# Turned tiles of a top-2 expert layer: dense 128-byte moves, rows one step sooner, weight loads on SyncE's queue, one flag per tile

## The chip, the cores and the metric

The kernel runs on one core of a Trainium2 chip. The metric is the device time of one execution in microseconds. The kernel before takes 1312.8 us (median of 3 runs, 1312.21 to 1313.14). A measurement of this kernel can tell a change from none at about 0.2%, some 2.6 us.

## What is computed

A retention-like attention feeds a dense feed-forward layer, and that feeds a layer of 8 experts of which every token takes two. The change touches the expert layer alone:

```python
logits = x @ w_gate
noise_scale = np.log1p(np.exp(x @ w_noise))
noisy_logits = logits + noise_scale * noise
top2 = np.argpartition(-noisy_logits, 2, axis=1)[:, :2]
# top2_w: softmax of the two
for e in range(E):                       # E = 8
    for k in range(2):
        mask = top2[:, k] == e
        h = np.maximum(x[mask] @ w1[e], 0.0)
        out[mask] += top2_w[mask, k, None] * (h @ w2[e])
```

x has 2304 rows of 512, w1[e] is 512x1024, w2[e] is 1024x512, all fp32.

## The kernel before

**Stages.** Attention and the dense layer take the first 500 us or so. During the dense layer the kernel writes, for every expert, a list of its tokens in DRAM. The expert layer then works through these lists in tiles of 128 tokens; in this run there are 41 tiles, 0 to 40, some five per expert. Which expert a tile belongs to is known only at run time: VectorE (DVE) computes two small tables, `tab` and `tab2`, with one column per tile, and every engine reads its numbers from there (`entry` and `entry2`, lines 358 and 362: a load of one value into a register, then register instructions).

**One tile g.** GpSimd (POOL) gathers its 128 rows of x (`xg`), two tiles in flight. They must be transposed for TensorE (PE), as must the hidden values between the two products. Tiles from 2 on are turned without TensorE: VectorE transposes blocks of 32x32 (`turn_x` into `turned_x`, `turn_hidden` into `hid`, in two halves h), and DMAs move each group of 32 partitions to its place (`move_x` into `x_there`, 4 moves of 64 KB; `move_hidden` into `h_there`, 2 times 4 moves of 64 KB). Each move writes 128 runs of 512 bytes. What lands has the elements of a column 4 apart, so that its readers step by 16 bytes (`landed`). ScalarE (ACT) makes the high part of every value (`split_moved`, with the Relu, and `split_moved_x`), VectorE the rest (`split_moved`, `split_moved_x`), since each product is done as three products of parts (`three`, lines 826 to 828).

**TensorE's order** is fixed: `expert_in(g + 1)`, then `expert_out(g)`, then `expert_in(g + 2)`, `expert_out(g + 1)`; each is 24 matmuls of 512 columns, and each waits for the lower parts that VectorE made.

**A step g of the others**, word by word in the code below: ScalarE waits for the rows of tile g+2, loads the row numbers of tile g+4 (`load_meta`), splits hidden(g), splits weights for tile g+1 (w1), splits x(g+2), splits weights for tile g (w2), loads raw weights twice (`load_weights`), and loads the row numbers of output tile g+1 (`next_rows`). VectorE makes the rest of hidden(g), turns x(g+2) and hidden(g+1), makes the rest of x(g+2), and adds the output of tile g (`add_output`). SyncE (SP) moves x(g+2), then hidden(g+1). GpSimd gathers rows of tile g+3 (`gather_x`), the old output rows of tile g (`old_rows`) and scatters the new ones (`send_rows`).

**Weights.** An expert's weights come in four quarters of 1 MB (`raw`), two of w1 and two of w2, and are split into `ew`, which holds two experts. The table says at which tiles a quarter is split (`T_SPLIT`) and loaded (`T_LOAD`): at an expert's first and second tile. So each `split_weights` asks two questions of the table and each `load_weights` two, by a load from `tab2` and a branch over what is left out. ScalarE asks eight times per step, VectorE four times.

**The loops** run over pairs of steps (`Fori`), so every engine jumps back once per two tiles.

## Time and profile of the kernel before

| | us |
|---|---|
| median of 3 runs | 1312.8 |
| the profiled execution | 1312.81 |
| span of its instructions | 1310.8 |
| TensorE busy (matmuls) | 1031.6 |
| VectorE busy | 563.7 |
| ScalarE busy | 446.6 |
| GpSimd busy | 206.6 |
| mean granted TensorE clock | 0.901 |

The page of the profile cuts the span into 40 slices. TensorE is over 90% busy in the first sixteen and between 40% and 80% in nearly all of the rest, which is the expert layer; no other engine is above 70% in any slice there. Starts are counted in us from the start of the span. "ACTq", "SPq", "DVEq" are the queues (sequencers) of these engines: register, branch and DMA-issuing instructions. "issue" is time in which an engine waited for nothing that the profile shows. The chain that ended last is followed back from the last instruction.

### The profile page before, as it was taken

To read this page: it belongs to the slowest core of one execution; us is meant where nothing else is said; L and a number is where in the kernel's file an instruction comes from. 1 tells how busy PE (TensorE), PEld (TensorE's weight loads), DVE (VectorE), ACT (ScalarE), POOL (GpSimd) and SP (SyncE) were. 2 spreads that over 40 slices of the span, in tenths; PEclk is the share of its full clock that TensorE was granted. 3 is DMA by queue.
4 is the path that set the end of the run, shared out by engine and by line. 5 is a ranking of instruction groups with operands and counts; after the bars stand their busy time and mean duration, and the time that the engine had idled before them with its cause. 6 is when DMAs were issued, how large, how long until landed. Compare 5 with 4: busy or idle time off the path is not lost.

```text
span 1310.8 us, 21213 instructions
## 1 busy us (share of the span) xinstructions
PE 1031.6 (79%) x5392; PEld 855.2 (65%) x5393; DVE 563.7 (43%) x919; ACT 446.6 (34%) x649; POOL 206.6 (16%) x198
## 2 busy tenths in 40 slices
PE   9999999999999999676777746665375577787764
PEld 8889989898989887555555635453354455565553
DVE  4665243333425466433333624464353444433342
ACT  2367555555555663111111311232232321111111
POOL 5500001010102023211122011100101112121111
PEclk9999999999999999788899878887778788878888
DMA  9835200000000532633333343344534333333331
GB/s 298 286 124 185 80 1 25 1 24 0 24 0 21 180 109 47 208 82 91 87 87 94 101 131 101 93 141 148 185 102 133 106 79 92 83 83 89 83 73 51
DMA packets 115285, 128.84 MB, mean 98 GB/s; under 512 B 26813, under 2 KB 91709, under 8 KB 111040
## 3 DMA queue, kind: packets, MB, share of 16 engines
q1 hardware_dynamic: 89472, 78.05, 21.0%
q0 software_dynamic: 10992, 27.84, 6.8%
q10 hardware_dynamic: 14688, 21.65, 5.1%
q14 instruction: 108, 0.88, 0.2%
q8 instruction: 25, 0.41, 0.1%
HBM read 81.31 MB, written 20.37 MB: 78 GB/s over the span
## 4 chain that ended last, share of the span: by engine, by line
PE 37%; ACTq 20%; issue 17%; DMA 7%; SPq 6%; DVE 5%; ACT 4%; DVEq 2%; POOL 0%; POOLq 0%
ACTq L362 11%; PE bank L826 11%; PE bank L828 10%; PE bank L827 10%; DMA x_there<-turned_x 6%; SPq L535 5%; ACTq L358 5%; DVE turned_x L1640 3%; ACT hT_hi L1237 3%; ACTq L375 2%; DVEq L362 2%; PE bank L776 1%; PE bank L750 1%; ACTq L379 1%; PE bank L769 1%
## 5 line engine op out<-in xcount | busy, mean ns | idle before, releaser
L826 PE MATMUL bank<-ew,hT_hi 128*128 (+1 forms) x320 | 154.1, 482 | 206.5 <-DVE hT_lo L1660 206.5
L826 PEld LDWEIGHTS bank<-ew,hT_hi 128*128 128x128 f32 x320 | 74.4, 232 | 238.4 <-issue 222.4
L1237 ACT ACTIVATE hT_hi<-h_there 128x512 fp32r<-128x512 f32 x76 | 80.2, 1103 | 353.7 <-issue 342.0
L1660 DVE SCALAR_TENSOR_TENSOR hT_lo<-h_there,hT_hi 128x512 fp32r<-128x512 f32 x76 | 79.0, 1069 | 279.6 <-ACT hT_hi L1237 279.6
L826 PE MATMUL bank<-ew,xgT_hi 128*128 (+1 forms) x328 | 138.6, 422 | 52.0 <-DVE xgT_lo L1654 47.5
L827 PE MATMUL bank<-ew,hT_hi 128*128 (+1 forms) x320 | 146.1, 456 | 0.0
L828 PE MATMUL bank<-ew,hT_lo 128*128 (+1 forms) x320 | 144.3, 451 | 0.0
L827 PE MATMUL bank<-ew,xgT_hi 128*128 (+1 forms) x328 | 134.3, 410 | 0.0
L828 PE MATMUL bank<-ew,xgT_lo 128*128 (+1 forms) x328 | 133.6, 407 | 0.0
L826 PE MATMUL bank<-xs_hi,mw 128*128 128x384 f32 x384 | 129.9, 338 | 0.0
L828 PE MATMUL bank<-xs_hi,mw 128*128 128x384 f32 x384 | 129.5, 337 | 0.0
L827 PE MATMUL bank<-xs_lo,mw 128*128 128x384 f32 x384 | 128.9, 336 | 0.0
L651 POOL DMA_INDIRECT out<-ysb,meta_y x41 | 42.9, 1047 | 534.6 <-DVE ysb L1673 534.6
L826 PEld LDWEIGHTS bank<-ew,xgT_hi 128*128 128x128 f32 x328 | 65.2, 199 | 81.3 <-issue 68.4
L1413 DVE SCALAR_TENSOR_TENSOR act_t<-bank,act_t 128x384 f32<-128x384 f32 x90 | 50.2, 558 | 150.7 <-ACT act_t L1153 149.8
L826 PE MATMUL bank<-mw,g_hi 128*128 128x512 f32 x288 | 114.6, 398 | 0.0
L828 PE MATMUL bank<-mw,g_lo 128*128 128x512 f32 x288 | 113.7, 395 | 0.0
L827 PE MATMUL bank<-mw,g_hi 128*128 128x512 f32 x288 | 113.4, 394 | 0.0
L1243 ACT ACTIVATE xgT_hi<-x_there 128x512 fp32r<-128x512 f32 x38 | 42.3, 1114 | 205.6 <-DMA x_there<-turned_x 205.6
L619 POOL DMA_INDIRECT lists<-rec,slot x36 | 35.6, 990 | 379.1 <-DVE slot L1512 370.0
L828 PEld LDWEIGHTS bank<-ew,hT_lo 128*128 128x128 f32 x320 | 73.3, 229 | 18.2
L827 PEld LDWEIGHTS bank<-ew,hT_hi 128*128 128x128 f32 x320 | 74.6, 233 | 15.8
(233 smaller groups left out, 1624.6 us busy)
## 6 DMA issues: line engine op xcount, KB each, us to landing
raw<-w_ex ACTq DMA_DIRECT2D x20, 1024.0 KB, 4.9
h_there<-hid SPq DMA_DIRECT2D x312, 64.0 KB
raw<-w_ex SPq DMA_DIRECT2D x12, 1024.0 KB, 5.1
x_there<-turned_x SPq DMA_DIRECT2D x152, 64.0 KB, 2.1
stage<-w_ff SPq DMA_DIRECT2D x16, 512.0 KB, 3.4
out<-blank SPq DMA_DIRECT2D x3, 1536.0 KB, 11.1
x_rows<-x2sb SPq DMA_DIRECT2D x6, 768.0 KB, 4.4
kbuf<-kN SPq DMA_DIRECT2D x16, 256.0 KB, 4.1
```

Of the source, the lines that this page charges most:

```text
L358: return eng.value_load(tab[row:row + 1, bass.ds(g, 1)], min_val=low, max_val=high)
L362: return eng.value_load(tab2[row:row + 1, bass.ds(g, 1)], min_val=low, max_val=high)
L535: sp.dma_start(x_there[:, i * P:(i + 1) * P], turned_x[32 * i:32 * i + 32, :].rearrange("a (j n) -> a j n", j=4)).then_inc(x_moved, 16)
L651: pool.indirect_dma_start(out=out[:, :], out_offset=rows, in_=ysb[:, s, :], in_offset=None, bounds_check=N - 1, oob_is_err=False).then_inc ...
L826: pe.matmul(o, a_hi, b_hi, start=first, stop=False)
L827: pe.matmul(o, a_hi, b_lo, start=False, stop=False)
L828: return pe.matmul(o, a_lo, b_hi, start=False, stop=last)
L1237: nc.scalar.activation(h_hi[:, 4 * h:4 * h + 4, :], landed(h_there[:, h, :]), ACT.Relu).then_inc(hT_hi_done, 1)
L1243: nc.scalar.activation(xgT_hi[:, s, :, :], landed(x_there[:, :]), ACT.Copy).then_inc(xgT_hi_done, 1)
L1413: dve.scalar_tensor_tensor(t, h_ps[f % 4], 0.0, t, ALU.max, ALU.add).then_inc(g_done, 1)
L1640: dve.transpose(turned_x[:, :].rearrange("p (j b c) -> p j c b", j=4, b=32), xg[:, s, :].rearrange("p (c a j) -> p j c a", j=4, a=32)).the ...
L1660: dve.scalar_tensor_tensor(h_lo[:, k, :], landed(h_there[:, h, :]), 0.0, as32(h_hi[:, k, :]), ALU.max, ALU.subtract).then_inc(hT_lo_done, 1)
```

## The change

Six edits, all in the expert layer.

- **Layout.** The turned tiles are laid out so that a move writes dense runs: `h_there` and `x_there` are now [128, tiles of 128 columns, 128], a move fills 32 of every 128 columns (runs of 128 bytes), and the readers read them without a step. VectorE's transposes write contiguous runs of 32.
- **Moves.** Hidden is moved in 4 moves of 128 KB (each 128 x 8 x 32) instead of 8 of 64 KB, after both halves are turned, under one semaphore. x is still moved in 4 of 64 KB (128 x 4 x 32).
- **Rows one step sooner.** VectorE turns x(g+3) at the end of step g, not x(g+2) near its beginning, and SyncE moves it behind hidden(g+1).
- **Weight loads** leave ScalarE's queue for SyncE's, behind the moves of the step.
- **One flag per tile** (`T_BUSY`, the larger of the two split flags): one question in front of each pair of splits and each pair of loads. The two questions behind it are asked only where the flag is set.
- **ScalarE's order.** Hidden(g) is split first, and the wait for rows and the load of row numbers come after.

```diff
-        h_there, a = place("h_there", [P, 2, 4 * P], F32, a)
-        x_there, a = place("x_there", [P, 4 * P], F32, a)
+        h_there, a = place("h_there", [P, FT2, P], F32, a)
+        x_there, a = place("x_there", [P, KT, P], F32, a)
...
-        def landed(ap):
-            return ap.rearrange("p (t c) -> p c t", c=4)
+        def landed(ap, i):
+            return ap[:, :, 32 * i:32 * i + 32]
...
-                    sp.dma_start(x_there[:, i * P:(i + 1) * P], turned_x[32 * i:32 * i + 32, :].rearrange("a (j n) -> a j n", j=4)
+                    sp.dma_start(landed(x_there, i), turned_x[32 * i:32 * i + 32, :].rearrange("a (n b) -> a n b", b=32)
...
-            def move_hidden(g, h):
-                sp.wait_ge(h_turned, g * 2 + h + 1)
+            def move_hidden(g):
+                sp.wait_ge(h_turned, g * 2 + 2)
                 for i in range(4):
-                    sp.dma_start(h_there[:, h, i * P:(i + 1) * P],
-                                 hid[32 * i:32 * i + 32, h * 512:(h + 1) * 512].rearrange("a (j n) -> a j n", j=4)
-                                 ).then_inc(h_moved[h], 16)
+                    sp.dma_start(landed(h_there, i), hid[32 * i:32 * i + 32, :].rearrange("a (n b) -> a n b", b=32)
+                                 ).then_inc(h_moved, 16)
...
+            def move(g, rows=True):
+                move_hidden(g + 1)
+                if rows:
+                    move_x(g + 3)
+                for of, p in (g + 1, 0), (g, 1):
+                    with sp.If(entry2(sp, T_BUSY, of, 0, 1)):
+                        load_weights(sp, of, p)
-            with sp.Fori(1, pair) as i:
+            with sp.Fori(1, prior) as i:
                 for s in range(2):
-                    g = 2 * i + s
-                    move_x(g + 2)
-                    move_hidden(g + 1, 0)
-                    move_hidden(g + 1, 1)
+                    move(2 * i + s)
+            move(2 * prior)
+            move(2 * prior + 1, False)
...
             def split_weights(g, p):
-                for q in range(2):
-                    with act.If(entry2(act, T_SPLIT[q], g, 0, 1)):
+                with act.If(entry2(act, T_BUSY, g, 0, 1)):
+                    for q in range(2):
+                        with act.If(entry2(act, T_SPLIT[q], g, 0, 1)):
...
             def step(i, s):
                 g = 2 * i + s
+                split_moved(g, g)
                 alone(act, got_x[s], i * 16 + 32)
                 load_meta(act, meta_x, s, g + 4, ld_mx[s])
-                split_moved(g, g)
                 split_weights(g + 1, 0)
                 split_moved_x(g + 2, s, g + 1)
                 split_weights(g, 1)
-                load_weights(act, g + 1, 0)
-                load_weights(act, g, 1)
                 next_rows(i, s)
...
-                dve.transpose(turned_x[:, :].rearrange("p (j b c) -> p j c b", j=4, b=32),
+                dve.transpose(turned_x[:, :].rearrange("p (j c b) -> p j c b", j=4, b=32),
...
+            dve.tensor_tensor(col(cols2, T_BUSY), other, goal, ALU.max)
...
             def step(i, s, end=False):
                 g = 2 * i + s
                 split_moved(g)
-                turn_x(g + 2, s, i + 2)
                 turn_hidden(g + 1, 0)
                 split_weights(g + 1, 0)
                 turn_hidden(g + 1, 1)
                 split_moved_x(g + 2, s)
                 split_weights(g, 1)
-                if end:
+                if not end:
+                    turn_x(1 - s, i + s + 2)
+                else:
                     split_moved(g + 1, hE_hi, hE_lo)
                 add_output(i, s)
```

SyncE's queue, kernel before: what stands at the top of its loop over pairs of steps, for the first of the two steps (x of tile g+2, then the two halves of hidden(g+1)).

```order
L561 ISA
L535 DMA x_there<-turned_x 128x1x128 [waits xgT_made]
L535 DMA x_there<-turned_x 128x1x128 x3
L540 ISA
L542 DMA h_there<-hid 128x1x128 [waits h_turned]
L542 DMA h_there<-hid 128x1x128 x3
L540 REGISTER_ALU
L542 DMA h_there<-hid 128x1x128 [waits h_turned]
L542 DMA h_there<-hid 128x1x128 x3
```

SyncE's queue, kernel after, the same place.

```order
L568 ISA
L541 DMA h_there<-hid 128x8x32 [waits h_turned]
L541 DMA h_there<-hid 128x8x32 x3
L532 REGISTER_ALU
L534 DMA x_there<-turned_x 128x4x32 [waits xgT_made]
L534 DMA x_there<-turned_x 128x4x32 x3
L361 ISA
L361 TENSOR_LOAD tab_116
L361 ISA x2
L565 COMPARE_AND_BRANCH
```

Hidden goes first and in half as many moves, x goes second, and behind them stand the flag's load and the branch over the weight loads.

ScalarE's queue, kernel before: from the jump target of its loop on (`hT_hi` is the high part of hidden, `tab_116` is `tab2`).

```order
L1330 ISA
L358 ISA [waits got_x0]
L358 TENSOR_LOAD tab
L358 ISA x2
L375 ISA
L375 DMA meta_x<-lists 128x2
L1236 REGISTER_ALU [waits m2_done]
L1237 ACTIVATE hT_hi<-h_there 128x512 [waits h_moved0]
L1237 ACTIVATE hT_hi<-h_there 128x512 [waits h_moved1]
```

ScalarE's queue, kernel after, the same place.

```order
L1334 ISA
L1241 REGISTER_ALU [waits m2_done]
L1242 ACTIVATE hT_hi<-h_there 128x512 [waits h_moved] x2
L335 ISA
L357 ISA [waits got_x0]
L357 TENSOR_LOAD tab
L357 ISA x2
L374 ISA
L374 DMA meta_x<-lists 128x2
```

The split of hidden stands ahead of the wait for rows.

VectorE's queue, kernel before: the end of one step (the output) and the beginning of the next.

```order
L1673 SCALAR_TENSOR_TENSOR ysb<-bank,meta_y,prev 128x512 [waits sent_y0,got_prev0]
L1658 ISA
L1660 SCALAR_TENSOR_TENSOR hT_lo<-h_there,hT_hi 128x512 [waits hT_hi_done]
L1658 REGISTER_ALU
L1660 SCALAR_TENSOR_TENSOR hT_lo<-h_there,hT_hi 128x512 [waits hT_hi_done]
L1640 STREAM_TRANSPOSE turned_x<-xg 128x4x4x32 [waits got_x1]
L1649 STREAM_TRANSPOSE hid<-bank 128x4x4x32 [waits in_half]
```

VectorE's queue, kernel after, the same place.

```order
L1644 STREAM_TRANSPOSE turned_x<-xg 128x512 [waits got_x1]
L1670 REGISTER_ALU
L1672 REGISTER_ALU [waits m2_done]
L1677 SCALAR_TENSOR_TENSOR ysb<-bank,meta_y,prev 128x512 [waits sent_y0,got_prev0]
L1662 ISA
L1664 SCALAR_TENSOR_TENSOR hT_lo<-h_there,hT_hi 128x512 [waits hT_hi_done]
L1662 REGISTER_ALU
L1664 SCALAR_TENSOR_TENSOR hT_lo<-h_there,hT_hi 128x512 [waits hT_hi_done]
L1653 STREAM_TRANSPOSE hid<-bank 128x4x128 [waits in_half]
```

The turning of x now stands ahead of the output of its step, and the turning of hidden follows its split directly.

## Rows read from the trace of the kernel before

**Rows 1.** Stretches of line L1237: us, ACT busy (count), PEclk, DMA share, GB/s
```profile
575.20:720.00 144.80, 16.89 (x16) 0.88 0.34 87
720.00:1083.20 363.20, 33.78 (x33) 0.80 0.41 120
1083.20:1294.90 211.70, 25.35 (x25) 0.87 0.33 83
```
**Rows 2.** Timeline of ACT: start, us, engine, line, names [idle before <-releaser]
```profile
1228.02 2.11 ACT L1237 ACTIVATE hT_hi<-h_there 128x512 fp32r<-128x512 f32 x2 [10.92 <-issue]
1236.44 1.12 ACT L1243 ACTIVATE xgT_hi<-x_there 128x512 fp32r<-128x512 f32 x1 [6.31 <-DMA x_there<-turned_x]
...
1244.30 2.12 ACT L1237 ACTIVATE hT_hi<-h_there 128x512 fp32r<-128x512 f32 x2 [6.74 <-issue]
```
**Rows 3.** Timeline of DVE, same step
```profile
1229.16 2.08 DVE L1660 SCALAR_TENSOR_TENSOR hT_lo<-h_there,hT_hi 128x512 fp32r<-128x512 f32 x2 [9.43 <-ACT hT_hi L1237]
1231.15 1.14 DVE L1640 STREAM_TRANSPOSE turned_x<-xg 128x512 f32<-128x512 f32 x1
1232.17 1.98 DVE L1649 STREAM_TRANSPOSE hid<-bank 128x512 f32<-128x512 f32 x2
...
1239.85 0.75 DVE L1673 SCALAR_TENSOR_TENSOR ysb<-bank,meta_y,prev 128x512 f32<-128x512 f32 x1 [1.18 <-issue]
```
**Rows 4.** Timeline of SP, same step
```profile
1232.32 2.48 SPq L535 DMA_DIRECT2D x_there<-turned_x  x4
1234.93 5.09 SPq L542 DMA_DIRECT2D h_there<-hid  x8
```
**Rows 5.** Timeline of PE: the first of each three matmuls
```profile
1218.43 0.69 PE L826 MATMUL bank<-ew,xgT_hi 128*128 x1 [2.68 <-DVE xgT_lo L1654]
1219.77 0.63 PE L826 MATMUL bank<-ew,xgT_hi 128*128 x1
...
1238.90 0.49 PE L826 MATMUL bank<-ew,xgT_hi 128*128 x1 [0.33 <-DVE xgT_lo L1654]
...
1243.78 0.39 PE L826 MATMUL bank<-ew,xgT_hi 128*128 x1
```
**Rows 6.** Pieces of the chain at the end of ACT's loop: start, us, what
```profile
1222.07 2.41 issue
...
1224.71 2.12 issue
```
**Rows 7.** Table loads of line L362 in 1228:1264.5: count: duration min/median/max in ns
```profile
L362 ACTq TENSOR_LOAD <-tab x16: 273/278/431, 1228.1 to 1256.5; - x16
```
**Rows 8.** Groups by form (busy us, mean ns), and a split of weights in ACT's timeline
```profile
L1257 ACT ACTIVATE ew<-raw 128x2048 f32 x24 | 45.9, 1914 | 38.7 <-issue 35.3 <-PE bank L828 3.4
L1833 DVE TENSOR_TENSOR ew<-raw,ew 128x2048 f32 x24 | 55.0, 2293 | 42.2 <-ACT ew L1257 42.2
...
963.81 1.92 ACT L1257 ACTIVATE ew<-raw 128x2048 f32 x1 [2.79 <-issue]
```
**Rows 9.** DMA queue 1 in 1230:1243 (moves): packets, MB, share of 16 engines
```profile
q1 hardware_dynamic: 1728, 0.79, 26.7%
```
**Rows 10.** DMA queue 1 in 63.05:63.85: mostly the gate weights' 128-byte runs
```profile
q1 hardware_dynamic: 573, 0.09, 74.7%
```
**Rows 11.** Issues of DMAs of many runs: duration min/median/max in ns
```profile
L477 SPq DMA_DIRECT2D wg<-w_gn x1: 1320/1320/1320, 61.1 to 61.1; - x1
...
L487 SPq DMA_DIRECT2D out<-blank x3: 636/1854/4470, 120.7 to 123.3; - x3
```
**Rows 12.** Instruction queue in 60.8:62.5, and an issue of 128 runs
```profile
q8 instruction: 1, 0.02, 4.4%
...
29.31 1.36 SPq L421 DMA_DIRECT2D qbuf<-qT  x1
```
**Rows 13.** Timeline of POOL
```profile
1224.63 1.01 POOL L645 DMA_INDIRECT prev<-out,meta_y  x1 [1.63 <-issue]
```
**Rows 14.** Page, part 6: gathers of old output rows, us to landing
```profile
prev<-out,meta_y POOLq DMA_INDIRECT x39, 3.4
```

66 lines of the change are left out of this document (33 added, 33 removed).

## The prediction, made before the changed kernel ran

> **What bounds the kernel now.** I read the two halves of the page first: only the expert layer has idle time on TensorE, so the question is what a step of it waits for. The stretches by the starts of ScalarE's split of hidden (two per tile) give the length of a step [rows 1]: 8 steps in 144.8 us and 12 in 211.7 us where no weights are split, together 356.5 / 20 = 17.8 us, and 16 steps in 363.2 us with the 24 quarters of weights (45.9 us at 1.91 [rows 8]). 363.2 - 16 x 17.8 = 78.4, or 3.3 us for each quarter.
>
> A step holds two products of 24 matmuls. At full clock one product runs from 1238.90 to the last triple at 1243.78 and ends 0.68 later: 5.56 us [rows 5]. Two take 11.1 us. So 6.7 of 17.8 us are waits. The timelines show whose. From 1228.02, where ScalarE splits hidden(g), the order is: VectorE's rest of hidden 2.08, turning of x 1.14, turning of hidden 1.98 [rows 3]; SyncE's eight issues for hidden begin only at 1234.93, behind the four for x, and end at 1240.02 [rows 4]; x is split at 1236.44, 1.6 us after the last issue for x had ended (1232.32 + 2.48 = 1234.80) [rows 2, 4]. By the same 1.6 us hidden(g+1) is there at 1241.6. But ScalarE takes it at 1244.30: since the end of x (1237.56) its queue has gone 6.74 us through questions to the table and two loads of row numbers [rows 2]. Sixteen questions are asked in two steps [rows 7]; six of the eight of a step stand in those 6.74 us, with two loads of row numbers, so that one costs about 0.7 us. In the other step of the pair ScalarE jumps back, and there it stands still for 2.41 and 2.12 us [rows 6]. Two limits lie close together, then: ScalarE's queue, and behind it the row VectorE, SyncE, ScalarE. TensorE has to slow down besides: after a wait of 2.68 us a triple takes 1.34 us (1218.43 to 1219.77), not 0.70 [rows 5], at the lower level of the clock.
>
> **The change, part by part**, for a step without weights.
>
> *ScalarE's questions and loads.* Eight questions become two, 6 x 0.7 = 4.2 us less per step. The four load questions and the waits for VectorE in front of weight loads go to SyncE. Hidden is split before the wait for rows and the load of row numbers, some 1.3 us, so these now lie under VectorE's work. Left on ScalarE after hidden: row numbers 1.2, question 0.7, x 0.6, question 0.7, row numbers 1.2; this is 4.4 us. The stall at the jump back, 4.5 us per pair, I keep: 9 us are under 11.1.
>
> *Dense reads.* Now 512 stepped columns take 1.06 us on ScalarE and 1.04 on VectorE [rows 2, 3]. Dense ones take 1914 / 2048 = 0.93 and 2293 / 2048 = 1.12 ns a column [rows 8], 0.48 and 0.57 us, with a fixed part about 0.6 and 0.65. In the row from hidden to hidden this is 0.45 + 2 x 0.4 = 1.2 us; bounds are 0 (if only the step of the write mattered) and 1.3. The Trainium skill, SBUF — State Buffer, Specifications and its note on cachelines, lets fp32 be stepped by up to 4 elements for free; by that the 1.2 us would not come, and the chain below would be 11.2 instead of 10.0. The rows speak against it, at double the time per column.
>
> *x one step sooner.* x(g+2) has landed before its step begins, so the 6.31 us that ScalarE waits for it [rows 2] go, and 1.14 of turning and 2.48 of issues leave the way of hidden [rows 3, 4]. Its rows must be gathered sooner by the same half step. They are asked for right after the output of the tile before is sent, a whole step ahead. I cost this at nothing. The turning now stands ahead of the output of its step and delays that if the gather is late; the old output rows stand ready at 1224.63 + 3.4 = 1228.0 for an addition at 1239.85 [rows 3, 13, 14], so 11.8 us of slack shrink to about 5.
>
> *Moves.* Four issues for hidden instead of eight. What one costs is not shown for this shape: 512-byte runs from 32 to 128 partitions took 2.48 / 4 = 0.62 us [rows 4], 512 runs of 128 bytes 1.32, 1536 runs of 1 KB 0.64 in the first of three [rows 11]. I take 0.62 to 0.7: the issue with 1.32 lies beside a transfer of instructions, and an issue of just 128 runs took 1.36 us elsewhere [rows 12], so 1.32 isn't the price of runs. The upper end is 1.32 for x and twice that for hidden. The data: 1728 packets of the moves took 26.7% of 16 engines for 13 us, 32 ns each [rows 9]; those of 128 bytes at most 0.747 x 800 x 16 / 573 = 16.7 ns [rows 10]. There are 4096 for hidden, 256 per engine, 4.3 us (1024 now, 64 per engine, 2.1 us, hidden behind the issues). At 32 ns it would be 8.2 us. I take 16.7, since that row has the size of the runs. So the transfers get slower, and the issues fewer: landing from the first issue about 1.1 + 4.3 + 0.5 = 5.9 us, against 5.09 + 1.6 = 6.7.
>
> *SyncE's weight loads.* At 1 MB each they queue behind the moves of their step and ahead of the next hidden, more than 8 us later. SyncE also waits there for VectorE's rest of the quarter, but x, in front of it, was turned behind both splits, so this wait is over. Behind it stands the next hidden. Nothing, while SyncE has 11.1 us and uses 2.5 + 2.5 + 1.4 plus its own jump back (bounded by ScalarE's 4.5).
>
> *The sum.* From the start of VectorE's rest of hidden(g): 1.4 + 1.98 turning + 5.9 landing + 0.6 split + 0.1 = 10.0 us to the same for g+1. TensorE needs 11.1, ScalarE 9 in the step with the jump. So TensorE becomes the bound, with handovers of 0.33 us [rows 5] twice: 11.7, and 0.2 for jumps that are not quite covered: 11.9 us. A quarter of weights keeps its 3.3 us: ScalarE's idle 2.79 and 1.92 [rows 8] are more than its slack of some 2 us, and VectorE's 2.29 stands between the halves of hidden as before; bounds 1.5 and 4.7. Then the three stretches: 144.8 - 8 x 11.9 = 49.6; 211.7 - 12 x 11.9 = 68.9; 363.2 - 16 x 11.9 - 24 x 3.3 = 93.6. The two steps ahead of them gain half as much each, 6. Together 218 us of the profiled 1312.8 (span 1310.8), which is the median of the runs: **1095 us**. The rest of the kernel gets one more operation on a table.
>
> **Rivals.** (1) *Jumps over the flagged blocks stall.* The block behind a flag is more than twice as long as those jumped over now, and the only long jumps of this trace cost 2.41 and 2.12 us [rows 6]. With two of these on ScalarE and on SyncE, SyncE has 2.5 + 2.5 + 1.4 + 2.2 + 4.4 = 13.0 us per step, with waits 14: 36 x 2.1 = 76 more, 1171. Against it: today's jumps of 17 instructions cost nothing that shows. The Trainium skill, Runtime: NRT & Kernel Launch, Instruction fetch mechanics, says that a taken branch to outside of a window of two pages stalls on a fetch; by its page size the flagged blocks would stay inside mostly, and the loop's jump would not.
>
> (2) *128-byte packets are as slow as the 512-byte ones*, 32 ns. The landing is 9.8, the chain 13.9: 36 x 2.0 = 72 more, 1167. The traffic of the moves has 32 ns where 128 bytes have 16.7 in a load from DRAM, and which of the two decides inside SBUF no row shows. The Trainium skill, DMA: Bandwidth & Descriptors, Specifications, has writes under 512 bytes done as read-modify-write, which speaks for this rival; its section Why small descriptors are slow (HBM only) excepts transfers within SBUF. The 128-byte row is such a write, and it shows no such price.
>
> (3) *Issues cost by runs: slower than before.* If SyncE needs 1.32 us for 512 runs and 2.64 for 1024, a step has 4 x 3.96 = 15.8, plus 1.4 and 2.3: 19.5 us of issuing on one queue, 1.7 more than now: 36 steps, 61 us, 1374. It turns into a loss from 3.5 us for both issues together. For it, the one row with 128-byte runs; against it, the 1536 runs in 0.64 us.
>
> (4) *It doesn't do what it says* in part: x comes sooner, but ScalarE still waits, for the rows or for output that is sent late. Half of the gain: 1204.
>
> **How the numbers follow.** Forecast 0.56, rival 1 0.14, rival 2 0.14, rival 3 0.06, rival 4 0.08, 0.02 for no difference at all. Only rival 3 and a part of the last give 0.06 slower; 0.02 within 0.2%, about what a measurement of this kernel can tell from no change; 0.92 faster. The low end has TensorE's 11.1 in all steps and 1.5 us for a quarter: 36 x 0.8 + 24 x 1.8 = 72 less, 1023; I take 1030. The high end takes in rivals 1 and 2 with their own spread: 1200.
>
> **What would show it.** Steps of 11.5 to 12.5 us without weights; the granted clock there near 1 where it was 0.87 and 0.88 [rows 1]; TensorE's gaps under 0.5 us; ScalarE with no wait on x; splits of hidden and x at 0.6 us on ScalarE. Issues for hidden at 0.6 to 0.7 (rival 3: 2.6), packets at 13 to 17 ns (rival 2: 32), waits of 2.2 us behind a flag (rival 1). The prediction is wrong if a step is bound by SyncE's queue, or if quarters of weights, whose price I only carried over, cost more once TensorE has no slack left.

## The result, and the profile after

The changed kernel takes **1076.6 us** (median of 4 runs, 1074.69 to 1077.91) where the kernel before takes 1312.5 (1310.44 to 1313.14) on the same chip: a ratio of 0.8204, 95% interval 0.8188 to 0.8219. The forecast was 1095, in a range of 1030 to 1200. The profiled execution has a span of 1074.8 us, 236.0 under that of before.

Page of the changed kernel: busy time by engine, two DMA queues (packets, MB, share of 16 engines), the chain by engine, and the split of hidden on ScalarE and VectorE.

```profile
PE 968.9 (90%) x5392; PEld 820.4 (76%) x5393; DVE 492.4 (46%) x920; ACT 389.4 (36%) x649; POOL 208.8 (19%) x198
...
q1 hardware_dynamic: 268032, 99.01, 36.0%
...
q14 instruction: 21, 0.17, 0.0%
...
PE 64%; SPq 9%; issue 8%; DMA 5%; ACTq 4%; DVE 4%; ACT 3%; DVEq 2%; POOLq 0%; POOL 0%
...
L1242 ACT ACTIVATE hT_hi<-h_there 128x512 fp32r<-128x512 f32 x76 | 43.8, 624 | 283.9 <-DMA h_there<-hid 283.9
...
L1664 DVE SCALAR_TENSOR_TENSOR hT_lo<-h_there,hT_hi 128x512 fp32r<-128x512 f32 x76 | 49.2, 689 | 79.0 <-ACT hT_hi L1242 49.5
```

The chain by engine and the instruction queue, kernel before:

```profile
PE 37%; ACTq 20%; issue 17%; DMA 7%; SPq 6%; DVE 5%; ACT 4%; DVEq 2%; POOL 0%; POOLq 0%
...
q14 instruction: 108, 0.88, 0.2%
```

PE has 64% of the chain, where it had 37%, and ScalarE's queue (ACTq) 4%, where it had 20%. ScalarE is idle for 284 us ahead of L1242, always for the moved hidden rows: it has become an engine that waits.

The stretches, by the starts of the split of hidden (L1242 now), for tiles 2 and 3, 4 to 11, 12 to 27 and 28 to 39; the columns are those of [rows 1].

```profile
539.40:564.60 25.20, 2.29 (x5) 0.88 0.73 175
564.60:654.60 90.00, 9.21 (x16) 1.00 0.68 140
654.60:926.30 271.70, 18.50 (x33) 0.89 0.64 159
926.30:1061.10 134.80, 13.78 (x24) 1.00 0.65 133
```

Against [rows 1]: the two stretches without weights (from here on "light" steps) go from 17.8 us a step to (90.0 + 134.8) / 20 = 11.24, at a granted clock of 1.00; the weight stretch goes from 363.2 to 271.7. With the light step taken off, a quarter of weights costs (271.7 - 16 x 11.24) / 24 = 3.8 us, where it was 3.3. The savings are 54.8 and 76.9 us in the light stretches, 91.5 in the weight stretch, and 12.8 at the two ends.

One light step of the changed kernel: ScalarE, then VectorE, then SyncE's issues (as [rows 2 to 4]).

```profile
1016.08 1.15 ACT L1242 ACTIVATE hT_hi<-h_there 128x512 fp32r<-128x512 f32 x2 [8.16 <-DMA h_there<-hid]
1016.99 0.34 ACTq L374 DMA_DIRECT2D meta_x<-lists  x1
1018.32 0.63 ACT L1248 ACTIVATE xgT_hi<-x_there 128x512 fp32r<-128x512 f32 x1 [1.09 <-DMA x_there<-turned_x]
1020.20 0.34 ACTq L374 DMA_DIRECT2D meta_y<-lists  x1
1026.71 1.15 ACT L1242 ACTIVATE hT_hi<-h_there 128x512 fp32r<-128x512 f32 x2 [7.75 <-DMA h_there<-hid]
```
```profile
1016.74 1.29 DVE L1664 SCALAR_TENSOR_TENSOR hT_lo<-h_there,hT_hi 128x512 fp32r<-128x512 f32 x2 [1.24 <-issue]
1017.95 0.71 DVE L1653 STREAM_TRANSPOSE hid<-bank 128x512 f32<-128x512 f32 x1
1020.51 0.72 DVE L1653 STREAM_TRANSPOSE hid<-bank 128x512 f32<-128x512 f32 x1 [1.85 <-PE bank L833]
```
```profile
1021.26 3.15 SPq L541 DMA_DIRECT2D h_there<-hid  x4
1024.63 2.64 SPq L534 DMA_DIRECT2D x_there<-turned_x  x4
```

The second half of hidden is turned when TensorE gives it ([1.85 <-PE bank]), the moves start at 1021.26, and the rows are there 5.45 us later, at 1026.71. ScalarE has waited 7.75 us for them. VectorE waits for TensorE, and TensorE stands still for no longer than 0.52 us in this stretch.

In the weight stretch that isn't so. Three of its waits, 654 to 926 us: engine, line, waited for; total us, times, longest.

```profile
PE bank L831 <- DVE xgT_lo L1658: 44.5, 11, 9.4
PE bank L831 <- DVE hT_lo L1664: 24.8, 8, 9.2
ACT ew L1263 <- DMA raw<-w_ex: 23.5, 3, 9.9
```

TensorE still stands for 69 us there, most of it for the low part of x. The experiments below mostly change this stretch.

### The profile page after: what moved, and what is told of

It reads as the page before. It is cut to its first block, busy times and chain, and to the rows that moved or that the text cites. A ratio compares the mean times of both kernels' runs of the same rounds, so it can differ in the third digit from the quotient of the medians.

```text
span 1074.8 us, 20634 instructions
## 1 busy us (share of the span) xinstructions
PE 968.9 (90%) x5392; PEld 820.4 (76%) x5393; DVE 492.4 (46%) x920; ACT 389.4 (36%) x649; POOL 208.8 (19%) x198
## 4 chain that ended last, share of the span: by engine, by line
PE 64%; SPq 9%; issue 8%; DMA 5%; ACTq 4%; DVE 4%; ACT 3%; DVEq 2%; POOLq 0%; POOL 0%
PE bank L831 19%; PE bank L833 19%; PE bank L832 19%; SPq L541 3%; DMA h_there<-hid 3%; SPq L361 2%; SPq L534 2%; ACT ew L1263 2%; ACTq L361 2%; PE bank L781 2%; DMA raw<-w_ex 1%; PE bank L755 1%; ACTq L357 1%; DVEq L361 1%; PE bank L774 1%
## 5 line engine op out<-in xcount | busy, mean ns | idle before, releaser
L831 PE MATMUL bank<-ew,xgT_hi 128*128 (+1 forms) x328 | 136.2, 415 | 49.3 <-DVE xgT_lo L1658 44.5
L831 PE MATMUL bank<-ew,hT_hi 128*128 (+1 forms) x320 | 130.0, 406 | 41.6 <-DVE hT_lo L1664 41.6
L1242 ACT ACTIVATE hT_hi<-h_there 128x512 fp32r<-128x512 f32 x76 | 43.8, 624 | 283.9 <-DMA h_there<-hid 283.9
L832 PE MATMUL bank<-ew,xgT_hi 128*128 (+1 forms) x328 | 132.9, 405 | 0.0
L833 PE MATMUL bank<-ew,hT_lo 128*128 (+1 forms) x320 | 127.7, 399 | 0.0
L832 PE MATMUL bank<-ew,hT_hi 128*128 (+1 forms) x320 | 127.6, 399 | 0.0
L656 POOL DMA_INDIRECT out<-ysb,meta_y x41 | 45.5, 1111 | 353.4 <-DVE ysb L1677 353.4
L831 PEld LDWEIGHTS bank<-ew,hT_hi 128*128 128x128 f32 x320 | 62.3, 195 | 59.3 <-issue 46.6
L1840 DVE TENSOR_TENSOR ew<-raw,ew 128x2048 f32 x24 | 55.0, 2293 | 94.2 <-ACT ew L1263 93.5
L1664 DVE SCALAR_TENSOR_TENSOR hT_lo<-h_there,hT_hi 128x512 fp32r<-128x512 f32 x76 | 49.2, 689 | 79.0 <-ACT hT_hi L1242 49.5
L1263 ACT ACTIVATE ew<-raw 128x2048 f32 x24 | 45.9, 1914 | 89.5 <-issue 53.4
L1154 ACT ACTIVATE act_t<-bank 128x384 f32<-128x384 f32 x90 | 44.1, 490 | 88.8 <-PE bank L833 82.6
```

The source lines that it names most:

```text
L656: pool.indirect_dma_start(out=out[:, :], out_offset=rows, in_=ysb[:, s, :], in_offset=None, bounds_check=N - 1, oob_is_err=False).then_inc ...
L831: pe.matmul(o, a_hi, b_hi, start=first, stop=False)
L832: pe.matmul(o, a_hi, b_lo, start=False, stop=False)
L833: return pe.matmul(o, a_lo, b_hi, start=False, stop=last)
L1154: nc.scalar.activation(t, h_ps[f % 4], ACT.Abs).then_inc(abs_done, 1)
L1242: nc.scalar.activation(h_hi[:, 4 * h:4 * h + 4, :], h_there[:, 4 * h:4 * h + 4, :], ACT.Relu).then_inc(hT_hi_done, 1)
```

## Experiments

Twelve kernels were run, each beside the kernel before (medians of 1310.1 to 1312.4 us). The table has the median, the ratio to before with its 95% interval, and three numbers from the profile of each, by the stretches above: us for a light step (tiles 4 to 11 and 28 to 39), for the weight stretch (12 to 27), and what a quarter of weights costs once 16 light steps are taken off.

| kernel | us | ratio | light | weights | quarter |
|---|---|---|---|---|---|
| before | 1312.5 | 1 | 17.8 | 363.2 | 3.3 |
| changed | 1076.6 | 0.8204 (0.8188-0.8219) | 11.24 | 271.7 | 3.8 |
| u1: changed, no flags | 1060.2 | 0.8074 (0.8040-0.8109) | 11.28 | 252.2 | 3.0 |
| u2: changed, loads on ScalarE | 1128.0 | 0.8602 (0.8584-0.8620) | 11.04 | 325.3 | 6.2 |
| u3: changed, old layout | 1067.9 | 0.8144 (0.8119-0.8170) | 11.31 | 264.9 | 3.5 |
| u4: changed, x late | 1100.2 | 0.8377 (0.8347-0.8408) | 11.96 | 279.4 | 3.7 |
| a2: before, loads on SyncE | 1101.2 | 0.8395 (0.8381-0.8409) | 13.20 | 253.5 | 1.8 |
| a5: before, x sooner | 1135.1 | 0.8651 (0.8637-0.8666) | 12.73 | 294.9 | 3.8 |
| a6: before, both of these | 1056.6 | 0.8064 (0.8049-0.8079) | 11.49 | 246.4 | 2.6 |
| i3: u1, x ahead of weights | 1076.2 | 0.8195 (0.8181-0.8208) | 11.54 | 268.3 | 3.5 |
| b1: i3, old layout | 1064.5 | 0.8107 (0.8091-0.8123) | 11.32 | 260.2 | 3.3 |
| c1: changed, no flags, old layout | 1055.4 | 0.8051 (0.8032-0.8071) | 11.31 | 251.9 | 3.0 |
| c2: c1, loads ahead of x | 1056.2 | 0.8053 (0.8032-0.8075) | 11.26 | 252.4 | 3.0 |
| c3: c2, loads later at the start | 1054.9 | 0.8053 (0.8034-0.8072) | 11.23 | 252.9 | 3.1 |

My theory was that ScalarE's queue had been the first limit of the kernel before and x in hidden's way the second, and that the changed kernel stands on TensorE with room on the other engines. The rivals: that the layout and the halved moves carried the gain, or the flags.

### One part undone in the changed kernel

**u1, no flags.** On ScalarE, VectorE and SyncE each block asks its own two questions again.

```
-                with act.If(entry2(act, T_BUSY, g, 0, 1)):
-                    for q in range(2):
-                        with act.If(entry2(act, T_SPLIT[q], g, 0, 1)):
+                for q in range(2):
+                    with act.If(entry2(act, T_SPLIT[q], g, 0, 1)):
...
-                    with sp.If(entry2(sp, T_BUSY, of, 0, 1)):
-                        load_weights(sp, of, p)
+                    load_weights(sp, of, p)
```

> The changed kernel with the common flag undone on ScalarE, VectorE and SyncE: each block of split or load asks its own two questions again (on ScalarE 4 a step where 2 are, on VectorE the same, on SyncE 4 where 2 are). Weight loads stay on SyncE. Theory S (slack: in the changed kernel TensorE bounds a light step at 11.2 us and ScalarE waits 6.3 us for the hidden rows there, so a part undone costs only what goes over its slack): 2 questions of 0.7 us are 1.4 us on an engine that waits 6.3 us, so nothing in a light step; 1076 to 1085 us. Rival F (the count of questions carried the gain): 1.4 us in each of 36 steps, 50 us, 1127 us. Rival C (the fetch stalls at the loop's end come with the size of the loop): the body keeps its size, so they stay away under this one too.

Measured: 1060.2 us, **16 us faster** than the changed kernel, which no theory had. Light steps are the same (11.28 and 11.24); all of it is in the weight stretch, 271.7 to 252.2 us. The flag asks one question instead of two where a block has nothing to do, and three instead of two where it has work. The first saving falls into light steps, which have room; the extra question falls into the steps in which TensorE waits. SyncE's issues in such a step show how large it is. First the changed kernel with the old layout (flags kept, u3), then the same without flags (c1), both around the start of tile 20:

```profile
774.74 2.49 SPq L534 DMA_DIRECT2D x_there<-turned_x  x4
780.52 7.33 SPq L378 DMA_DIRECT2D raw<-w_ex  x3
791.28 2.68 SPq L541 DMA_DIRECT2D h_there<-hid  x4
```
```profile
770.39 2.50 SPq L534 DMA_DIRECT2D x_there<-turned_x  x4
775.41 6.44 SPq L378 DMA_DIRECT2D raw<-w_ex  x3
786.18 2.66 SPq L541 DMA_DIRECT2D h_there<-hid  x4
```

From the end of x to the first raw quarter: 780.52 - 777.23 = 3.29 with the flag, 775.41 - 772.89 = 2.52 without. And 7.33 against 6.44 for the three loads, between which the second flag stands. Together 1.7 us on SyncE alone in one step; ScalarE and VectorE ask theirs in the same steps. On SyncE this does not delay the move of hidden here: from the end of the loads to its first issue SyncE has 3.4 us with the flag (787.85 to 791.28) and 4.3 without (781.85 to 786.18). It makes the loads later. So the runs show that the flag costs 16 us; that it costs them by its extra questions is argued from their size, and how they divide among the three engines was not tried.

**u2, weight loads back on ScalarE**, behind its splits, with the flag.

```
                 split_weights(g, 1)
+                for of, p in (g + 1, 0), (g, 1):
+                    with act.If(entry2(act, T_BUSY, of, 0, 1)):
+                        load_weights(act, of, p)
                 next_rows(i, s)
...
-                for of, p in (g + 1, 0), (g, 1):
-                    with sp.If(entry2(sp, T_BUSY, of, 0, 1)):
-                        load_weights(sp, of, p)
```

> The changed kernel with the weight loads back on ScalarE's queue at the end of its step, behind the common flag. Theory S: 2 questions (1.4 us) and the stalls at the loop's end (2.4 + 2.1 us a pair, should the longer body bring them back) fit in the 6.3 us that ScalarE waits for the hidden rows; nothing in light steps, some us in the 24 quarters: 1077 to 1095 us. Rival Q (ScalarE's queue is still what sets the step): 1.4 + 2.3 us in each of 36 steps, 1210 us. Rival C: the queue-instruction fetches go from 21 packets of 8192 B back to about 108 and the stalls at the loop's end return, whatever the total does.

Measured: 1128.0 us, 51 more. The upper theory had 1077 to 1095, the rival 1210, so both missed; only rival C, that the fetches come back, holds (128 packets). Light steps don't get longer (11.04), as the slack has it. Queue 14 on the page of u2, and ScalarE in the weight step of tile 20, as an example:

```profile
q14 instruction: 128, 1.05, 0.3%
```
```profile
829.15 6.86 ACTq L378 DMA_DIRECT2D raw<-w_ex  x3
836.89 0.34 ACTq L374 DMA_DIRECT2D meta_y<-lists  x1
837.35 1.15 ACT L1239 ACTIVATE hT_hi<-h_there 128x512 fp32r<-128x512 f32 x2 [9.91 <-issue]
```

Issuing three quarters takes ScalarE 6.86 us, questions included, and the split of hidden stands behind it. A quarter costs 6.2 us instead of 3.8. The weight stretch is 53.6 us longer; the light steps and the time ahead of tile 2 give back 4 each, tiles 2 and 3 and the end take 4 more, and that is the 50 by which the spans differ. TensorE's wait for the low part of hidden in the weight stretch goes from 24.8 to 60.8 us. I had carried the slack of light steps (6.3 us) over to weight steps. ScalarE does wait for hidden there too, 102.8 us in 16 steps of the changed kernel, but unevenly: 11.19 us ahead of the split at 708.22 and 1.51 ahead of that at 806.01, where quarters crowd.

**u3, the old order of elements**: runs of 512 bytes, reads with a step of 4, four moves kept.

```
...
-                    sp.dma_start(landed(h_there, i), hid[32 * i:32 * i + 32, :].rearrange("a (n b) -> a n b", b=32)
+                    sp.dma_start(h_there[:, :, i * P:(i + 1) * P], hid[32 * i:32 * i + 32, :].rearrange("a (j u n) -> a j u n", j=4, u=2)
...
-                    nc.scalar.activation(h_hi[:, 4 * h:4 * h + 4, :], h_there[:, 4 * h:4 * h + 4, :], ACT.Relu
+                    nc.scalar.activation(h_hi[:, 4 * h:4 * h + 4, :], landed(h_there[:, h, :]), ACT.Relu
...
-                dve.transpose(hid[:, :].rearrange("p (j u c b) -> p j u c b", j=4, u=2, b=32)[:, :, h, :, :],
+                dve.transpose(hid[:, :].rearrange("p (j u b c) -> p j u c b", j=4, u=2, b=32)[:, :, h, :, :],
...
```

> The changed kernel with the old order of elements within a row of the moves: runs of 512 B and reads with a step of 4 elements by ScalarE and VectorE; the number of moves (4 for hidden, 4 for x) is kept. Theory S: both transposes +0.65 us, each split +0.45 us, in the chain of the hidden rows some 2 us, against a slack of 1 to 2 us: light steps 11.2 to 12.5, total 1077 to 1115 us. Rival L (the layout carried the gain, with the packets): each of 36 steps +3 us or more, 1180 us and up. If the 128-byte packets cost more in the changed kernel than the 512-byte ones, this run comes out faster than it, under 1074 us.

Measured: 1067.9 us, **9 us faster**, which is the case of the last sentence above. The operations did get slower, as the page of u3 shows:

```profile
L1242 ACT ACTIVATE hT_hi<-h_there 128x512 fp32r<-128x512 f32 x76 | 81.1, 1115 | 259.2 <-DMA h_there<-hid 259.2
...
L1664 DVE SCALAR_TENSOR_TENSOR hT_lo<-h_there,hT_hi 128x512 fp32r<-128x512 f32 x76 | 79.3, 1073 | 63.8 <-ACT hT_hi L1242 60.6
```

1115 ns for 624, 1073 for 689, and the turning of hidden 1084 for 712. In light steps that is covered (11.31), and the sum over all steps still falls, so the moves must pay more for dense runs than the readers gain. DMA queue 1 in 939:1050, of the changed kernel and of u3, and then all hidden issues of the two in that stretch (ns min/median/max):

```profile
q1 hardware_dynamic: 63559, 7.97, 44.6%
```
```profile
q1 hardware_dynamic: 16226, 7.68, 29.5%
```
```profile
L541 SPq DMA_DIRECT2D h_there<-hid x40: 617/672/1734, 943.1 to 1046.1; - x40
```
```profile
L541 SPq DMA_DIRECT2D h_there<-hid x40: 616/625/685, 943.9 to 1047.0; - x40
```

A packet takes 0.446 x 111 x 16 / 63559 = 12.5 ns in the changed kernel and 0.295 x 111 x 16 / 16226 = 32.3 ns in u3. These are means over all packets of the queue, and each move has 16 of 4 bytes among them (in the packed trace, 9.0 ns each); without them it is 12.5 ns for 128 bytes and 34.2 for 512: cheaper each, but half as much again for the same bytes. And issues of 1024 runs now and then stand still for up to 1.73 us, which those of 256 runs don't. The difference is largest behind raw loads: the first hidden move after the start takes 6.68 us of issuing in the changed kernel (at 529.00) and 4.52 in u3. Tile 4 begins 4.9 us sooner in u3, of which 1.2 us are there before the first move (the raw loads ahead of it begin at 524.14 and 522.95), and the weight stretch is 6.8 us shorter. Whether the issues or the packets make the 9 us was not tried apart.

**u4, x turned and moved one step later**, as before.

```
                 split_moved(g)
+                turn_x(s, i + 2)
                 turn_hidden(g + 1, 0)
...
-                if not end:
-                    turn_x(1 - s, i + s + 2)
-                else:
+                if end:
...
+                    move_x(g + 2)
                     move_hidden(g + 1)
-                    move_x(g + 3)
```

> The changed kernel with x turned and moved one step later, as before: VectorE turns x of the tile after next between the splits and the hidden halves of the same step, and SyncE issues x ahead of hidden. Flags, layout, halved moves and loads on SyncE stay. Theory S: 1.1 us of turning and 2.5 us of issues return in the way of the hidden rows, and ScalarE waits again for x; the hidden chain goes from 10.0 to about 13.5 us over TensorE's 11.1: 36 steps x 2.4 us, 1140 to 1190 us, the costliest single part. Rival Q (ScalarE's queue alone had been the limit, x was in nobody's way): under 1095 us.

Measured: 1100.2 us, 24 more: between the two ranges. The light step is 11.96 us, not 13.5. The chain through late x is only 0.9 us over TensorE's floor of 11.1, where I had 2.4. A likely reason, not tried, is that the hidden issues behind x are four here and not eight and that what the chain passes is faster. The sign was right and the size off by a factor of three.

### One part added to the kernel before

With room everywhere, undoing says little on what lifted the kernel. So parts were added singly to the kernel before.

**a2, weight loads on SyncE**, no flags, nothing else.

```
                 split_weights(g, 1)
-                load_weights(act, g + 1, 0)
-                load_weights(act, g, 1)
...
                     move_hidden(g + 1, 1)
+                    load_weights(sp, g + 1, 0)
+                    load_weights(sp, g, 1)
```

> The kernel before with one part added: the weight loads on SyncE behind the moves instead of on ScalarE, no flags, nothing else. ScalarE's questions go from 8 a step to 4. Theory Q (ScalarE's queue was the first limit of the kernel before, x in the way of hidden the second): 2.8 us of questions and the stalls at the loop's end (2.3 us a step) go, then the late x and the 12 moves bound at 14 to 15 us a light step (17.8 before): 1150 to 1210 us. Rival X (x in hidden's way was the first limit): hardly anything, 1280 to 1312 us. Queue-instruction fetches fall from 108 to about 20 packets if the loop's length on ScalarE is what brings them.

Measured: 1101.2 us: **this one part, alone, gives 211 us**, where the whole change gives 236. The light step goes from 17.8 to 13.20 us, the quarter from 3.3 to 1.8, both better than the range I had given (14 to 15 us, 1150 us and up). ScalarE in a light step, and queue 14:

```profile
1004.51 2.13 ACT L1239 ACTIVATE hT_hi<-h_there 128x512 fp32r<-128x512 f32 x2 [3.53 <-issue]
1012.91 1.11 ACT L1245 ACTIVATE xgT_hi<-x_there 128x512 fp32r<-128x512 f32 x1 [6.28 <-DMA x_there<-turned_x]
```
```profile
q14 instruction: 18, 0.15, 0.0%
```

The wait on x is still there with 6.28 us; hidden is taken as soon as ScalarE comes to it. The instruction fetches are gone (18 for 108), and the stalls with them.

**a5, x one step sooner**, nothing else: VectorE's turn_x at the end of the step, SyncE's move_x(g + 3) behind both halves of hidden, twelve moves, the old layout.

```
-                turn_x(g + 2, s, i + 2)
...
+                if not end:
+                    turn_x(1 - s, i + s + 2)
...
-                    move_x(g + 2)
                     move_hidden(g + 1, 0)
                     move_hidden(g + 1, 1)
+                    move_x(g + 3)
```

> The kernel before with one part added: x turned and moved one step sooner, behind the hidden halves, nothing else (12 moves a step, old layout, ScalarE keeps the loads and its 8 questions, no flags). Theory Q: the wait of 6.3 us on x goes, but ScalarE's own row of work is 8 x 0.7 of questions, 3.3 of splits, 1.4 + 0.7 of list loads and 2.3 of stalls, 13 us a step at least: light steps 13.5 to 16, 1180 to 1260 us. Rival X (x was the first limit, ScalarE had room): light steps at 12 or under, 1110 to 1150 us.

Measured: 1135.1 us, below my range and inside the rival's (1110 to 1150), though the light step of 12.7 us is above the 12 that the rival had. What is left of it is ScalarE's queue all the same. ScalarE in two light steps of a5, and queue 14:

```profile
1018.42 2.11 ACT L1245 ACTIVATE hT_hi<-h_there 128x512 fp32r<-128x512 f32 x2 [11.18 <-issue]
...
1027.86 1.11 ACT L1245 ACTIVATE hT_hi<-h_there 128x512 fp32r<-128x512 f32 x1 [6.31 <-issue]
...
1044.69 1.11 ACT L1245 ACTIVATE hT_hi<-h_there 128x512 fp32r<-128x512 f32 x1 [11.25 <-issue]
```
```profile
q14 instruction: 109, 0.88, 0.2%
```

ScalarE waits for nobody ahead of hidden ("issue"): it is in its own questions and fetches for 11.2 us in the step with the jump back and for 6.3 in the other. The pair shown takes 1044.69 - 1018.42 = 26.3 us, and all light steps but the last two 13.0 each in the mean, which is what I had counted as ScalarE's own work at the least; the last two, without a jump, bring the mean in the table to 12.73.

Taken together a2 and a5 say more than that both matter. Of a light step of the kernel before, 17.8 us, the queue alone takes off 4.6 and x alone 5.1. Both of my theories spoke of a first and a second limit, of which the second would stand once the first was gone, and both forecasts were too high. The rows show one ring instead. From the split of hidden at 1228.02 to the next at 1244.30 the chain of the kernel before passes without a gap through the turning of x (1231.15), its issues (1232.32 to 1234.80), its split (1236.44 to 1237.56) and then ScalarE's 6.74 us of questions and row numbers [rows 2 to 4]. In a ring the parts add up, and what is taken from either shortens it, until TensorE's 11.1 us bound the step; 4.6 and 5.1 are together more than the 6.6 that the change could take off.

**a6, both of these** on the kernel before.

```
...
+            def move(g, rows=True):
+                move_hidden(g + 1, 0)
+                move_hidden(g + 1, 1)
+                if rows:
+                    move_x(g + 3)
+                load_weights(sp, g + 1, 0)
+                load_weights(sp, g, 1)
...
```

> The kernel before with two parts added and nothing else: weight loads on SyncE, x one step sooner. It keeps the 12 moves, the old layout, no flags, the old order on ScalarE. Theory Q (these two lift the kernel to TensorE's bound, the rest of the change is worth nothing or less): light steps 11.1 to 11.6, total 1050 to 1070 us, under the changed kernel's 1076. Rival M (halving the moves matters once the queue is free: 8 hidden issues of 0.6 us and two separate waits): light steps 12 to 13, 1080 to 1100 us.

Measured: **1056.6 us, 20 under the changed kernel**, ratio 0.8064 against 0.8204, with intervals far apart. Light steps 11.49, the weight stretch 246.4, the shortest of all. So two parts of the change carry all of its gain. Flags, layout, halved moves and ScalarE's new order together cost 20 us on top of them. In light steps they do bring 0.25 us (11.49 to 11.24), 5 us in twenty. Of the four it is the flags and the layout that cost: c1 below has the other two and not these, and at 0.8051 (0.8032 to 0.8071) it is the same as a6.

### Looking for a better one

**i3, x ahead of the weights** in both rows, from u1.

```
+                split_moved_x(g + 2, s, g + 1)
                 split_weights(g + 1, 0)
-                split_moved_x(g + 2, s, g + 1)
...
                 turn_hidden(g + 1, 0)
-                split_weights(g + 1, 0)
                 turn_hidden(g + 1, 1)
                 split_moved_x(g + 2, s)
+                split_weights(g + 1, 0)
```

> The changed kernel without the common flag (the run of 1060 us), and on ScalarE the split of the moved x ahead of the weights' block, on VectorE both halves of the turned hidden rows and the split of x ahead of it. Theory W (in weight steps TensorE waits, 37 us for the low part of x and 15 us for the low part of hidden, because these stand in line behind weights that nobody needs yet): most of the 37 and some of the 15 go: 1020 to 1045 us, light steps unchanged at 11.0 to 11.2. Rival D (the weight steps are set by the raw loads on SyncE and the DMA engines, which the hidden rows share): 1055 to 1062, the waits only move to the hidden rows.

Measured: 1076.2 us, 16 slower than u1, and slower than either theory had. TensorE's idle time by what ended it, over the whole run, u1 and then i3:

```profile
L830 PE MATMUL bank<-ew,xgT_hi 128*128 (+1 forms) x328 | 136.9, 417 | 40.9 <-DVE xgT_lo L1656 37.0
...
L830 PE MATMUL bank<-ew,hT_hi 128*128 (+1 forms) x320 | 130.4, 408 | 27.3 <-DVE hT_lo L1662 27.3
```
```profile
L830 PE MATMUL bank<-ew,hT_hi 128*128 (+1 forms) x320 | 135.2, 423 | 65.8 <-DVE hT_lo L1662 65.8
...
L830 PE MATMUL bank<-ew,xgT_hi 128*128 (+1 forms) x328 | 132.1, 403 | 22.1 <-DVE ew L1837 18.6
```

The wait for x went, 37.0 us. In its place TensorE waits 18.6 us for the weights themselves, which I had taken for work that nobody needs yet, and 38.5 us more for hidden.

**b1, the old layout on i3** (both edits are shown above).

> As the run with x ahead of the weights, and with the old order of elements (512-byte runs, stepped reads), 4 + 4 moves. Theory P (the 128-byte packets cost SyncE's issues and the DMA engines more than dense reads give the engines, seen as -8.8 us when the layout alone was undone): 5 to 10 us under the run beside it, 1012 to 1040 us. Rival R (the two gains are the same wait, or ScalarE and VectorE have less room now): the same or slower than the run beside it by up to 10 us.

Measured: 1064.5 us, above its range because i3 was, but 11.7 under i3: the gain of u3 a second time, in another order of work. Ratios 0.8107 and 0.8195, intervals apart.

**c1, no flags and the old layout** (u1 and u3 together).

> The changed kernel with both parts undone that each made it faster when undone alone: no common flag (-16 us alone) and the old order of elements with 512-byte runs (-9 us alone). Theory N (the flag costs questions in the weight steps, the 128-byte runs cost SyncE's issues, both on the way to the same steps but separate pieces of it): the gains add up to most of 25 us, 1048 to 1056 us. Rival O (one and the same wait in the weight steps): 1057 to 1062 us, no better than without flags alone.

Measured: 1055.4 us, 21 less than the changed kernel: the upper edge of what adding up would give. It is 4.8 us under u1, whose interval overlaps, and 12.5 under u3, whose interval does not. So the flag's cost shows in either layout, and the layout's cost is shown with flags (u3) and in i3's order (b1), but not on u1.

**c2, weight loads ahead of x** on SyncE, from c1.

```
                 move_hidden(g + 1)
+                for of, p in (g + 1, 0), (g, 1):
+                    load_weights(sp, of, p)
                 if rows:
                     move_x(g + 3)
-                for of, p in (g + 1, 0), (g, 1):
-                    load_weights(sp, of, p)
```

> As the run beside it (no flags, old layout), and SyncE's weight loads behind the hidden moves and ahead of the moves of x, which are needed only a step later. Theory D (in the weight stretch ScalarE waits for raw quarters whose loads stand behind the turn and the four issues of x: 2.5 us of issues and 1 to 3 us until x is turned, in each step with a load): raw quarters land 3 to 5 us sooner in about 12 steps with loads, 1020 to 1045 us, light steps as they were. Rival E (the time goes to the splits themselves and the hidden moves behind the raw loads in the queue): within 4 us of the run beside it.

Measured: 1056.2 us, as the rival had it: no difference. The steps of tiles 19 and 21 became shorter than in c1 (17.92 us for 20.50, 16.25 for 21.96), those of 14, 16 and 20 longer (16.79 for 15.12, 12.29 for 10.09, 23.12 for 20.05); the stretch stays at 252.

**c3, raw loads later at the start**: SyncE issues the moves for tiles 2 to 4 ahead of raw quarters, from c2.

```
-            load_weights(sp, 0, 0)
-            load_weights(sp, 1, 0)
             sp.wait_ge(x2_stored, 16 * NCH)
...
             move_hidden(2)
             move_x(4)
...
+            load_weights(sp, 0, 0)
+            load_weights(sp, 1, 0)
+            move_hidden(3)
...
```

> As the run with loads ahead of x (1056 us), and at the start of the moved steps the raw quarters for later experts are issued behind the moves of hidden and x for tiles 2, 3 and 4 and not ahead of them. Theory V (two raw loads take 4.6 us of SyncE's issues ahead of the first hidden move and 5.8 ahead of the second, and ScalarE waits 12.7 and 10.2 us for these rows; TensorE waits with it): first hidden rows 4 to 5 us sooner, the step for tile 4 begins at about 551 to 555 us of the trace where it was 560.0; 1046 to 1052 us. Rival T (the rows were not turned sooner anyway, or TensorE has other things late there): tile 4 at 557 to 560, within 3 us of the run before.

Measured: 1054.9 us, no difference. The cause I named was there, and taking it away moved the wait. ScalarE's first splits, c2 and then c3:

```profile
535.70 1.11 ACT L1241 ACTIVATE hT_hi<-h_there 128x512 fp32r<-128x512 f32 x1 [12.71 <-DMA h_there<-hid]
```
```profile
526.39 1.15 ACT L1246 ACTIVATE hT_hi<-h_there 128x512 fp32r<-128x512 f32 x1 [2.66 <-DMA h_there<-hid]
...
545.98 1.11 ACT L1246 ACTIVATE hT_hi<-h_there 128x512 fp32r<-128x512 f32 x1 [14.04 <-DMA h_there<-hid]
...
556.48 1.11 ACT L1252 ACTIVATE xgT_hi<-x_there 128x512 fp32r<-128x512 f32 x1 [8.39 <-DMA x_there<-turned_x]
```

Hidden(2) is there 9.3 us sooner. Then hidden(3) waits 14.04 us, its issues behind two raw loads, and x(5), behind two more, 8.39. Tile 4 begins at 559.9, as in c2 at 560.0.

## Why the prediction was right, point by point

**What bounds it.** Right: TensorE. Light steps at 11.24 us stand 0.1 over the floor of 11.1 that [rows 5] gave, at full clock. The forecast of 11.9 held two handovers of 0.33 us and 0.2 for jumps; these terms were too large. The gaps are covered, and the longest in 1010:1040 is 0.52 us. That is 0.66 x 20 = 13 us of the 18 by which the forecast was high. Another 4.6 us are the two first steps, which gained 10.6 and not 6, and 2.2 the end. In the weight stretch the two errors cancel: 16 x 0.66 = 10.6 us too much for steps and 24 x 0.53 = 12.7 too little for quarters, 271.7 measured and 269.6 forecast. That this stretch came out within 2.1 us is luck.

**ScalarE's queue first, x second.** Right that both bound the step, wrong that they were two limits with an order. With the queue relieved alone (a2) the light step is 13.2 and ScalarE waits on x; with x relieved alone (a5) it is 12.7, even less, and ScalarE is in its own queue nearly all the time; with both (a6) it is 11.5. They were parts of one ring, as said at a5. It did no harm to the forecast, since the change relieves both. What the prediction did not ask is whether the rest was needed.

**The stall at the jump back, 4.5 us a pair, "I keep".** Wrong. Queue 14 carried 108 packets before and 21 after. The loads on ScalarE bring them and take them: 18 and 19 without (a2, a6), 109 and 128 with (a5, u2). So a2's 4.6 us per step are four questions (2.8) and about half of a 4.5 us stall, 5.0 by that count. In light steps of the changed kernel the error cost nothing: u2 has the fetches and steps of 11.04. ScalarE's 9 us in the step with the jump also left out the split of hidden itself, 1.15 us; 10.1 would still have been under 11.1.

**Dense reads, 0.6 and 0.65 us.** The durations are right (0.62 and 0.69). The hidden turning also fell, from 0.99 to 0.71 each, which was not in the sum. The step of this chain that failed is its value: 1.2 us in a chain that is 1.1 us under the bound are worth nothing, and the prediction's own sum of 10.0 against 11.1 said so. The Trainium skill, SBUF — State Buffer, says two things here: its note on cachelines lets fp32 be stepped by up to 4 elements for free, and its Specifications ask for at least two hits in each line of 16 bytes, of which such a step gives one. The runs agree with the second and not with the first: 1115 against 624 ns for the same 512 columns.

**Moves.** Hidden's issues at 0.67 us (forecast 0.62 to 0.7), packets at 12.5 ns (16.7), landing 5.45 us after the first issue (5.9). All near. Not foreseen: what more runs do to SyncE behind raw loads. The choice of four moves with 128-byte runs loses to four with 512-byte runs by 9 us (u3) and 12 (b1 on i3); without flags the 4.8 us from u1 to c1 are not clear of noise.

**x one step sooner.** Right in its worth; alone it gives 177 us on the kernel before, and undone in the changed one it costs 24. The wait of 6.31 us is gone. But x does not land before its step begins, as the prediction had it: its moves queue behind hidden's, and the last of their packets starts at 1028.66 (in the packed trace), 2 us after the split of hidden at 1026.71 and 0.35 ahead of the split of x at 1029.01. The 1.15 us that stand ahead of that split are filled by ScalarE's load of row numbers and its question, so x comes just in time here.

**The flag.** The sum counted it in light steps only, six questions less on ScalarE. Four of the six were the moved loads, and the other two bring nothing there. In a step with work the flag is a third question, and this term was missing. Without the flag the kernel is 16 us faster and a quarter costs 3.0 us instead of 3.8.

**Weight loads on SyncE cost nothing.** Right for light steps. In weight steps they delay hidden: the four issues at 822.05 took 5.57 us behind three quarters that took 7.28. But on ScalarE they cost 51 us more (u2).

**A quarter of weights, 3.3 us, bounds 1.5 to 4.7.** It became 3.8, inside the bounds, so by its own sign the prediction is wrong in this term. It named lack of slack as what could go wrong; u1, at 3.0, says that the flag does it, since without it a quarter costs less than the 3.3.

**The rivals.** Rival 1 (jumps over flagged blocks stall): no wait of 2.2 us is seen in a light step; between hidden and x ScalarE needs 1.09 us. Rival 2 (32 ns a packet): 12.5 measured, so it is out. Four packets of 128 bytes take 50 ns where one of 512 takes 34, so small ones have a price. Its ground in the Trainium skill, DMA: Bandwidth & Descriptors, Specifications, is that writes under 512 bytes are done as read-modify-write; the section gives no price for it, and no run here shows that this is the cause. A fixed part of each packet would do as well, since those of 4 bytes take 9.0 ns. Rival 3 (1.32 us and 2.64): 0.67 and 0.63, so it is out, though single issues of 1.73 us occur. Rival 4: in light steps ScalarE doesn't wait for x beyond its own 1.1 us. It is out too.

**Still open.** What sets the weight stretch at about 252 us in u1, c1, c2 and c3, and at 246 in a6. Its parts (x, hidden, raw quarters, the splits themselves) give way to one another: i3 and c2 each took one away and another took its place. And why a6, with eight moves in two halves, is 5 us shorter there than c1 was not tried; in total time the two can't be told apart.

## What to carry to other kernels

Once the likely bound is a full engine, ask of each part of a change whether it is still needed: here two parts (a queue relieved, a transfer started one step sooner) gave all of the gain. Of four more, each with a good reason of its own, the flags and the dense layout took 20 us back and the halved moves and the new order gave nothing that shows. Before ranking limits, look whether they lie on one ring: there each part counts, and none has to go first. A flag over a block saves a question where there is room and adds one where there is work, so count it in the steps that wait. And slack belongs to a kind of step: that of light steps (6 to 8 us on ScalarE) did not cover the steps with weights, where putting the loads back on ScalarE cost 51 us.

## What the runs showed of the hardware

- Stepped reads by 4 elements cost ScalarE 1115 ns for 512 fp32 columns where dense ones cost 624, and VectorE 1073 where 689. VectorE's turning of a PSUM bank into SBUF takes 712 ns with dense runs of 32 written (changed kernel, 939:1050) and 1085 in the old order (u3, the same stretch); the same operation from SBUF (x) takes 1081 and 1084 there.
- Within SBUF a packet of 4 bytes takes 9.0 ns, one of 128 bytes 12.5, one of 512 bytes 34.2 in the mean (changed kernel and u3, 939:1050). Four moves with 1024 runs each land 5.45 us after the first issue.
- Issues of 1024 runs mostly cost SyncE what those of 256 cost (672 and 625 ns in the median), but up to 1734 ns singly, and 6.68 us for four behind two loads of 1 MB where those with longer runs took 4.52.
- Whether ScalarE's loop stalls on instruction fetches followed the weight-load code in it: 108 to 128 packets on the instruction queue with it (before, a5, u2), 18 to 21 without (a2, a6, the changed kernel, u1). Whether the length of the loop or the branches in it do this was not tried apart.
